# Attention, gated MLP and soft mixture of experts in one kernel: four edits around the last stage (loading, order of the softmax over tokens, filler products, mixing)

## What is computed

```
q, k, v: 4 x 8 x 576 x 64;  f: 4 x 8 x 576                       (batch, heads, tokens, head width)
attn = softmax(q k^T / 8 + cum(log f)_i - cum(log f)_j, causal) v
x    = attn, heads side by side: 2304 tokens x 512
h    = x @ w_in  (512 x 2048);   x = (h * sigmoid(1.702 h)) @ w_out  (2048 x 512)
logits     = x @ phi                                             (2304 x 32 slots)
d          = softmax of logits over the tokens (axis 0)
slot_input = d^T @ x                                             (32 x 512)
for e in range(8):                                               (4 slots of each expert)
    slot_out[4e:4e+4] = relu(slot_input[4e:4e+4] @ w1[e]) @ w2[e]   (w1: 512 x 1024, w2: 1024 x 512)
c          = softmax of logits over the slots (axis 1)
out        = c @ slot_out                                        (2304 x 512)
```

## Time and profile before

| | us |
|---|---|
| runs | 795.5, 800.78, 802.11 |
| median | 800.78 |
| the profiled execution, own time | 800.72 |
| its span (first to last instruction) | 798.9 |

### The profile page before, as it was taken

How to read it: one execution, slowest core, us unless ns; L and a number is a source line. 1 busy time by engine, 2 the same in 40 slices (tenths; PEclk the granted TensorE clock), 3 DMA queues, 4 the chain that set the end, 5 groups by cost and what they waited for, 6 DMA issues and landing times.

```text
span 798.9 us, 15703 instructions
## 1 busy us (share of the span) xinstructions
PE 737.5 (92%) x5993; PEld 692.3 (87%) x5993; DVE 504.6 (63%) x1387; ACT 370.7 (46%) x903; POOL 394.3 (49%) x427
## 2 busy tenths in 40 slices
PE   3999889999999989999999989999998999997986
PEld 3888789999998979999998989999998899993652
DVE  5899968768768656676768367777663444424313
ACT  4777855455557264546455354646432122111113
POOL 4344355564656465666565264747454476520000
PEclk9999989999999999999999899999999999997995
DMA  4434313334132323333333123332223345489976
GB/s 99 102 98 114 102 29 96 84 91 112 55 91 83 98 78 88 87 97 91 91 90 91 34 58 91 91 92 81 66 70 102 117 134 196 138 311 357 405 294 237
DMA packets 96507, 96.65 MB, mean 121 GB/s; under 512 B 61297, under 2 KB 61297, under 8 KB 96433
## 3 DMA queue, kind: packets, MB, share of 16 engines
q1 hardware_dynamic: 96432, 95.66, 39.2%
HBM read 90.84 MB, written 4.79 MB: 120 GB/s over the span
## 4 chain that ended last, share of the span: by engine, by line
PE 70%; DVE 16%; ACT 5%; issue 4%; DMA 3%; POOL 2%; SPq 0%; POOLq 0%; ACTq 0%; DVEq 0%
PE mb L1142 47%; PE yb L1022 5%; PE xb L1068 4%; PE zb L1041 4%; DMA ring_b<-in_moe_w 2%; DVE ptl L813 2%; DVE prob L807 2%; PE mb L1080 2%; ACT prob L658 2%; DVE xl L824 1%; DVE kl L775 1%; PE xb L1002 1%; DVE qs L771 1%; PE zb L1238 1%; PE mb L1182 1%
## 5 line engine op out<-in xcount | busy, mean ns | idle before, releaser
L1142 PE MATMUL mb<-xh,wih 128*128 128x288 f32 x512 | 160.8, 314 | 15.5 <-DVE hid L890 10.9
L1142 PE MATMUL mb<-gh,woh 128*128 128x288 f32 x512 | 157.9, 308 | 5.2 <-DVE x2t L897 4.0
L617 POOL TENSOR_TENSOR gl<-hid,gh 128x288 fp32r<-128x288 f32 x128 | 115.5, 909 | 83.8 <-ACT gh L700 82.6
L1142 PE MATMUL mb<-xh,wil 128*128 128x288 f32 x512 | 152.7, 298 | 0.0
L1142 PE MATMUL mb<-xl,wih 128*128 128x288 f32 x512 | 152.7, 298 | 0.0
L1142 PE MATMUL mb<-gl,woh 128*128 128x288 f32 x512 | 151.0, 295 | 0.0
L1142 PE MATMUL mb<-gh,wol 128*128 128x288 f32 x512 | 151.0, 295 | 0.0
L890 DVE SCALAR_TENSOR_TENSOR hid<-gate,mb 128x288 f32<-128x288 f32 x128 | 57.9, 453 | 119.3 <-ACT gate L706 118.2
L634 POOL TENSOR_TENSOR wol<-stage,woh 128x512 fp32r<-128x512 f32 x64 | 82.4, 1288 | 90.3 <-DVE woh L765 90.3
L658 ACT ACTIVATE prob<-prob,m_row 64x576 f32<-64x576 f32 (+4 forms) x160 | 96.5, 604 | 58.8 <-DVE m_row L793 58.4
L634 POOL TENSOR_TENSOR wil<-stage,wih 128x512 fp32r<-128x512 f32 x64 | 82.6, 1290 | 72.1 <-DVE wih L765 72.1
(11 more groups left out here) (160 smaller groups left out, 1443.8 us busy)
## 6 DMA issues: line engine op xcount, KB each, us to landing
stage<-in_moe_w_in SPq DMA_DIRECT2D x64, 256.0 KB, 3.0
stage<-in_moe_w_out SPq DMA_DIRECT2D x64, 256.0 KB, 2.7
ring_a<-in_moe_w SPq DMA_DIRECT2D x16, 1024.0 KB, 8.1
ring_b<-in_moe_w SPq DMA_DIRECT2D x14, 1024.0 KB, 11.4
cum_b<-cum_dram SPq DMA_DIRECT2D x32, 288.0 KB, 3.7
qk_in<-in_q SPq DMA_DIRECT2D x32, 144.0 KB, 3.0
qk_in<-in_k SPq DMA_DIRECT2D x32, 144.0 KB, 3.5
v_in<-in_v SPq DMA_DIRECT2D x32, 128.0 KB, 3.2
```

The costliest lines, as they stand in the source:

```text
L617: pool.tensor_tensor(gl[:, i % FT, HALF * (i // FT):HALF * (i // FT + 1)], hid[:, i % RING, :], gh[:, i % FT, HALF * (i // FT):HALF * (i / ...
L1142: ins = mm(bank[:, 0:HALF], a[:, t, P * (j % 4):P * (j % 4) + P], x[:, t, cols], start=(i == 0), stop=(i == 11))
```

## The change

Four edits. **Memory:** in the MLP's memory `stage`, `hid` and `gate` move ahead of `woh`, with a gap behind them, so that ring place 6 lies over `wil`'s end, `stage`, `hid`, `gate` and the gap, and no longer over `woh` and `wol`; piece 6 is loaded when the last weight split and the last `gl` are done, and 7 and 8 still at the end of the units. **Order:** the dispatch moves ahead of the sums' product, so `t_pe` 3 is now the dispatch (SP waits for it before piece 9) and `t_pe` 4 the sums; the transposes of the last, 64-row tile (`turn_last(4)`) move behind the transpose of `gmax`; on DVE several small steps move (below). **Filler:** `busy(n)` issues n products of 128 columns of `ident_r` with itself into a bank that nobody reads, 7 behind `turn_last(4)` and 16 behind the spreading product. **Mixing:** the 20 products go to all eight banks in turn, and the outputs get 20 places of their own in `ring_a` 0 to 2, so that no copy waits for a transfer.

```
+        stage = sb("stage", [P, 2, QF], F32, mlp_mem)
+        hid = sb("hid", [P, RING, HALF], F32, mlp_mem)
+        gate = sb("gate", [P, RING, HALF], F32, mlp_mem)
+        sb("gap", [P, 256], F32, mlp_mem)
         woh = sb("woh", [P, FT, MODEL], F32R, mlp_mem)
         wol = sb("wol", [P, FT, MODEL], F32R, mlp_mem)
-        stage = sb("stage", [P, 2, QF], F32, mlp_mem)
         gh = sb("gh", [P, FT, SEQ], F32R, mlp_mem)
         gl = sb("gl", [P, FT, SEQ], F32R, mlp_mem)
-        hid = sb("hid", [P, RING, HALF], F32, mlp_mem)
-        gate = sb("gate", [P, RING, HALF], F32, mlp_mem)
...
+                    sp.wait_ge(w_lo, BATCH * 32)
+                    sp.wait_ge(g_lo, BATCH * 32 + RING)
+                    load_expert(6)
                     sp.wait_ge(unit_done, m * U_MLP + U_MLP)
-                    for e in range(6, NR - 1):
+                    for e in range(7, NR - 1):
...
-            sp.wait_ge(t_pe, 4)
+            sp.wait_ge(t_pe, 3)
             load_expert(NR - 1)
...
+            def busy(n):
+                for _ in range(n):
+                    mm(mb[:, 1, 0:P], ident_r[:, :], ident_r[:, :], start=True, stop=True)
...
             tr(zb[0:SLOTS, 0, 0:P], gmax[:, :], ident[:, :]).then_inc(t_pe, 1)
+            turn_last(4)
+            busy(BUSY[0])
             pe.wait_ge(t_dve, 3)
             mm(zb[:, 1, 0:SLOTS], ones[0:SLOTS, :], dmax[:, :], start=True, stop=True).then_inc(t_pe, 1)
+            busy(BUSY[1])
+            pe.wait_ge(t_act, 1)
+            pe.wait_ge(t_dve, 4)
+            pe.wait_ge(token_out, 1 + BATCH * QT)
...
+            for t in range(nt):
+                ins = dispatch(t)
+            ins.then_inc(t_pe, 1)
             pe.wait_ge(t_dve, 6)
...
-                if t >= NOUT:
-                    act.wait_ge(out_dma[t % NOUT], 16 * (t // NOUT))
-                nc.scalar.copy(obuf[:, t % NOUT, :], zb[:, 0, :]).then_inc(mixed_out[0], 1)
+                nc.scalar.copy(obuf[t], mix_ps[t % 8]).then_inc(mixed_out[0], 1)
...
-                if t >= 2:
-                    pe.wait_ge(mixed_out[t % 2], t // 2)
-                mm(zb[:, t % 2, :], ct4[:, t, :], so4[:, :], start=True, stop=True).then_inc(mixed, 1)
+                if t >= 8:
+                    pe.wait_ge(mixed_out[t % 2], t // 2 - 3)
+                mm(mix_ps[t % 8], ct4[:, t, :], so4[:, :], start=True, stop=True).then_inc(mixed, 1)
```

More of the change, by code:

```diff
@@ L66 @@
 RING = 4
+BUSY = (7, 16)
 INV_SQRT_D = DIM ** -0.5
@@ L333, in build @@
         NR = len(ring)
-        obuf = ring_a[0][:, :].rearrange("p (i n) -> p i n", i=NOUT)
+        obuf = [ring_a[t // 8][:, MODEL * (t % 8):MODEL * (t % 8) + MODEL] for t in range(NOUT)]
         cum_dram = nc.dram_tensor("cum_dram", (BATCH * HEADS, SEQ), F32).ap()
@@ L358, in build @@
         e_dma = [sem(f"e_dma{i}") for i in range(NR)]
-        out_dma = [sem(f"out_dma{i}") for i in range(NOUT)]
+        out_dma = sem("out_dma")
         const_made = sem("const_made")
@@ L565, in _ @@
                 sp.wait_ge(mixed_out[t % 2], t // 2 + 1)
-                sp.dma_start(out[SEQ * b + P * i:SEQ * b + P * i + QW[i], :], obuf[0:QW[i], t % NOUT, :]
-                             ).then_inc(out_dma[t % NOUT], 16)
-            for i in range(NOUT):
-                sp.wait_ge(out_dma[i], 16 * ((BATCH * QT - 1 - i) // NOUT + 1))
+                sp.dma_start(out[SEQ * b + P * i:SEQ * b + P * i + QW[i], :], obuf[t][0:QW[i], :]).then_inc(out_dma, 16)
+            sp.wait_ge(out_dma, 16 * BATCH * QT)
         @block.gpsimd
@@ L909, in _ @@
             nc.vector.tensor_reduce(gmax[:, :], gm[:, :, :].rearrange("p b s -> p s b"), AX_X, ALU.max).then_inc(t_dve, 1)
-            nc.vector.memset(x2last[64:P, 4, :], 0.0)
-            for i in range(4):
-                ins = nc.vector.tensor_copy(sel4[32 * i:32 * i + 32, :], ident[32 * i:32 * i + 32, 32 * i:32 * i + 32])
-            ins.then_inc(sel_made, 1)
             dve.wait_ge(t_pe, 1)
@@ L922, in _ @@
                                     ALU.subtract).then_inc(t_dve, 1)
-            dve.wait_ge(token_out, 1 + BATCH * QT)
-            nc.vector.memset(mb[:, :, 0:256], 0.0)
-            nc.vector.memset(yb[:, 0, 0:P], 0.0)
+            for i in range(4):
+                ins = nc.vector.tensor_copy(sel4[32 * i:32 * i + 32, :], ident[32 * i:32 * i + 32, 32 * i:32 * i + 32])
+            ins.then_inc(sel_made, 1)
             dve.wait_ge(t_act, 1)
```

44 lines of the change are left out of this document (23 added, 21 removed).

## The result

The changed kernel takes 794.29 us in the median of 20 runs (789.74 to 799.04), the kernel before 799.71 us on the same chip. The ratio is 0.9937, 95% interval 0.9920 to 0.9954, so 5.0 us (3.7 to 6.4) are gained. The forecast was 796.5 us, its range 792.4 to 799.5, and "within 1%" had 0.82: the time lies in the range and the gain within 1%. But the sum got there by two terms that are off in opposite directions, and the case that came true for the dispatch is one that I had not taken as the likeliest: that the two errors nearly cancel is luck. Of the 2.2 us between 796.5 and 794.29, 1.1 come from the kernel before alone, whose median is 799.71 here and was 800.78 in the three runs that I started from. The rest of this document is about the terms.

The account below looks back on a forecast made before the run. Up to the mixing, weight transfers were taken as the bound, following the dispatch's end, with PE's limit 1.6 us below. 800.72 - 0 (third place) - 0.5 (head) - 3.7 (mixing) = 796.5 us, range 792.4 to 799.5.

Parts of the forecast that it names:

- Third ring place: Loading piece 6 earlier fills 4.4 us of idle transfers, which return ahead of piece 9; gain 0.
- the high clock: Rival: clock high through fillers and dispatch, which ends at 730.9, 4.0 us earlier; total 793.0 us, chance 0.32.
- the head: The stretch ahead of the mixing, up to and behind the dispatch: gain between -0.1 and +4.0 us, taken as 0.5.
- The chain to the dispatch: Steps from `gmax` through fillers and dispatch: dispatch ends 0.1 us later at low clock, 4.0 earlier at high clock.
- the low clock: Case the forecast started from: clock low through the fillers, dispatch starts at 729.1 and ends at 735.0, 0.1 us later.
- My sign of being wrong: Prediction wrong if fillers begin and end inside the waits with the clock at 1.00, or outputs stay near 300 GB/s.
- Everything up to the mixing shifts one for one with the end of the dispatch: Pieces 9 to 15 follow the dispatch without a hole, 37 us, as long as PE keeps up.
- Behind the dispatch: Sums' product, `den` and `rden` now precede `part`: PE's limit moves 0.9 us less, transfers still decide; cost nothing.
- The mixing: Final products and outputs: with eight banks, outputs at 400 GB/s take 11.8 us, 15.1 in all instead of 19.0; gain 3.7.
- The rival with 355 GB/s: Mixing: outputs leave at about 355 GB/s, gain there 2.3 us; total 797.9 us, chance 0.12.
- The third place's rival: Loading piece 6 earlier pays after all with the clock high: gain 5.8 + 3.7, total 791.2 us, chance 0.05.
- the slower one: Rival: clock stays low through dispatch and up(0), PE's limit 7.3 us later; total 802.7 us, chance 0.06.

Follow-up runs that it names:

- e2: The kernel before with the memory moved and piece 6 loaded with the last first-layer unit, nothing else changed; ratio to the kernel before 0.9982.
- e3: The changed kernel without the third ring place: piece 6 loaded at the end of the units again, memory still moved; ratio to the kernel before 0.9932.
- e5: The changed kernel with piece 9 loaded once the first 8 of the dispatch's 20 tiles are done; ratio to the kernel before 0.9914.
- e9: The changed kernel, unaltered, timed and profiled a second time; ratio to the kernel before 0.9940.
- e10: e5 again, unaltered, beside e9 on the same chip; ratio to the kernel before 0.9896.
- e11: e5 without the 23 filler products; ratio to the kernel before 0.9926.
- e1: The kernel before with only the mixing changed, to eight banks and 20 output places; ratio to the kernel before 0.9967.
- e7: The changed kernel with the changes of e5 and e6 together; ratio to the kernel before 0.9897.
- e6: The changed kernel with 10 more filler products behind the sums' product and 4 behind the product that adds the groups; ratio to the kernel before 0.9909.
- e8: e7 with pieces 8 and 7 loaded in the other order; ratio to the kernel before 0.9914.
- e12: The changed kernel with eight banks in the mixing but only the 8 output places of the kernel before; ratio to the kernel before 0.9923.
- e4: The changed kernel without its 23 filler products; ratio to the kernel before 0.9945.

## Why the prediction was right, and where it was not

**Third ring place, 0 on its own.** Right, by e2. The forecast's words that the idle time comes back ahead of piece 9 hold as well: e2 has its hole there. But I had the term at 0 "in each sum below but one rival's", and for the high clock that is wrong by my own rows: without the place the transfers run on to 735.2 whatever the head does, and a shorter head can close only the hole from there to 736.6, 1.4 us. The other 2.6 of that rival's 4.0 need the place. e3 shows the first half of this: down(7) starts 1.5 us earlier than before, with the dispatch 3.1 earlier and no hole left. The second half came only in part, 0 to 1.3 us.

**The chain to the dispatch: -0.5, bounds -0.1 and +4.0.** Here the likeliest case was the wrong one. I took the low clock, and the rival with the clock high through fillers and dispatch (0.32) came true: it put the dispatch at 8.1 to 12.9 us behind the units (726.1 to 730.9), and it is 8.16 to 12.66. Of the difference, 0.3 us is the dispatch itself, priced at 4.8 us with a spacing of 0.445 and 0.35 of latency for which I named no row; it takes 4.50, its ten groups 0.43 us apart. The step that failed is "in the only trace at hand the clock is low on this whole stretch, so I start from the low end". What one trace shows of the clock is one draw: in the profiles of kernels with the old order it falls at 721.6, 725.3 and 726.0, and the fillers change the draw itself (nine of nine with the dispatch at 1.00). PE's idle time of 3.2 us ahead of the dispatch was in my rows, and the filler that replaces it was the reason to start from the other end. My sign of being wrong, fillers that begin and end inside the waits with the clock at 1.00, came half true: the clock was at 1.00, and the fillers ran 0.5 and 0.2 us over the waits.

**"Everything up to the mixing shifts one for one with the end of the dispatch."** This is the step that was wrong in every case of mine. The dispatch ends 4.1 us earlier, down(7) starts only 1.55 and 2.83 us earlier. From the issue of piece 9 to down(7) it takes 42.6 and 41.4 us instead of 40.0. The runs show three parts of this; how much each of them costs is not separated. First, piece 10's issue: it hangs on up(0), so on everything between dispatch and up(0). Sums, `den` and `rden` now stand in there (0.6 us), and in the first profile the low clock (1.4 us), so that it follows piece 9's by 6.3 us instead of 4.3; piece 9 keeps the transfers busy for 5.2. In e5, where the lag is 7.5, the hole ahead of piece 10 is the only one. Second, the transfers themselves, which move less after the third place and where piece 10 begins (e9: 243 GB/s over 2 us), and whose last engines come late: 110 and 200 GB/s in the last 4 us, 242 before. Third, PE's own limit, 1.8 us below (1.68 in e9), which e10 and e11 reach. So even the right clock case would have given me 793.0, below the 794.3 measured.

**Behind the dispatch, 0.9 later for PE.** The measured steps: from the dispatch's end to up(0) 3.21 us (12.66 to 15.87) and 3.01 in e9, against 2.42 before: 0.6 to 0.8. Right in size. But I priced it on PE's limit only, and its first effect was on piece 10's issue.

**The mixing, -3.7.** Right in kind, too large: 3.07 and 2.63 in the changed kernel, 3.05 in e1. The supply is as forecast: transfers start 2.1 us behind the first product (2.3), and nothing moves in the last 0.9 us. The term that was mis-sized is the transfers' own: 11.8 us by bytes, plus 0.2 for the 64-row tiles, where 12.9 us are measured. At 405 GB/s the 16 full tiles take 10.4 us; that leaves 2.5 us, or 0.6 for each of the four half tiles, as much as a full one. The windows agree: 315 GB/s where the fifth output leaves, 248 where the tenth does, with the share at 0.97 to 1.01. The kernel before shows such an output by itself, as its fifth goes out behind a pause; its 16 engines are all busy, at half the rate of a full one:

```profile
785.50:786.00 0.50, 0.50 (x2) 0.21 (x1) 0.08 (x1) 0.24 (x1) 0.00 (x0) 0.50 1.00 221
```

That all four half tiles account for the whole of the 2.5 us follows from these windows; no run changed the tile. The rival with 355 GB/s was near the rate (364 measured); its gain of 2.3 us and the forecast's 3.7 have the measured ones between them.

The Trainium skill ("DMA: Bandwidth & Descriptors", Where 436 GB/s comes from), with its limit of about 358 GB/s, would have given 13.2 us, as the estimate in the prediction has it, near the 12.9 measured. The traces bear out the time and not the rule: the outputs go at 405 GB/s for 2.7 us, and the loads at 404 to 408 for 30 to 50 us.

**The sum.** 4.2 us were forecast and 5.0 measured: the head brought 1.5 to 2.8 instead of 0.5, the mixing 2.6 to 3.1 instead of 3.7. Two errors of 1.7 and 0.85 us, with opposite signs, which luck let nearly cancel. The third place's rival and the slower one did not come; the slower one needed a low clock through dispatch and up(0) with fillers, which no profile shows.

**A version that is likely ahead of both.** The ratios of e7, e5 and e10 are 0.9897, 0.9914 and 0.9896, 2 to 3.5 us below the changed kernel's 0.9937 and 0.9940. But e6, without the early piece 9, has 0.9909. Over the five profiles with it (e5, e7, e8, e10, e11) down(7) starts 53.8 us behind the units in the mean, over the five without (changed, e9, e12, e6, e4) 55.1. So the semaphore that lets piece 9 go when its eight tiles have been read is the likely reason, at the edge of what these runs resolve.

## What to carry to other kernels

When a step ahead of a row of transfers gets shorter, follow each later issue to its own release as well: a gain passes on one for one only while every next issue comes sooner than the piece ahead of it is through, and here the second issue was already within 1 us of that. Wait for what a transfer overwrites, not for the whole step that also reads other things. And treat the clock in one trace as one draw: look at what the engine does ahead of the stretch, before and after the change, and give the case that the change itself favours the larger chance.
